# Inverting softmax sums as 128x9 through DRAM, dealing the feed-forward's first steps anew, and storing weight blocks early

## The reference

```python
scores = q @ k.T / 8
bias = -(cum[:, :, :, None] - cum[:, :, None, :])       # cum = cumsum(max(s, 0))
scores = where(causal, -1e9, scores + minimum(bias, 0))
attn = exp(scores - max); attn = attn / (sum(attn) + 1e-9)
x = attn @ v                                            # heads side by side: 576 x 512
h = maximum(x @ w_in, 0)                                # 576 x 1024
conv = three taps along the sequence, per channel
x1 = (h * sigmoid(conv)) @ w_out                        # 576 x 512
u = x1 + (x1.T @ U @ V).T                               # rank 32
out = u + maximum(u @ w_ch1, 0) @ w_ch2                 # 512 -> 2048 -> 512
```

## Time and profile before

| what | value |
|---|---|
| median of three runs | 1002.07 us |
| the profiled execution's own time | 999.37 us |
| its span in the profile | 997.6 us |
| mean granted TensorE clock | 0.971 of full |
| TensorE (PE) busy, matmuls | 929.6 us, 93% |
| VectorE (DVE) busy | 531.9 us, 53% |
| ScalarE (ACT) busy | 350.8 us, 35% |
| DMA queue q1 | 154.66 MB, 49.9% of 16 engines' span |
| chain of work that ended last | PE 75%, DVE 13%, ACT 3%, issue 3%, DMA 2%, SP's issuing 2% |

### The profile page before, as it was taken

How to read it: one execution, slowest core, us unless ns; L and a number is a source line. 1 busy time by engine, 2 the same in 40 slices (tenths; PEclk the granted TensorE clock), 3 DMA queues, 4 the chain that set the end, 5 groups by cost and what they waited for, 6 DMA issues and landing times.

```text
span 997.6 us, 16111 instructions
## 1 busy us (share of the span) xinstructions
PE 929.6 (93%) x6455; PEld 868.0 (87%) x6455; DVE 531.9 (53%) x913; ACT 350.8 (35%) x670; POOL 5.9 (1%) x20
## 2 busy tenths in 40 slices
PE   2898898979999899999999999999999989999998
PEld 1676788968999799987999999987999989889998
DVE  5459896346775583346554784146655670342222
ACT  1365564444333443433332453332332331211111
POOL 1000000000000000000000000000000000000000
PEclk9799997989999799999999999999999999999999
DMA  4677455735564646533645546433555434344441
GB/s 93 137 213 189 110 165 171 214 101 157 179 205 153 180 127 211 191 120 129 186 163 170 169 130 207 154 112 113 177 169 169 170 127 162 127 136 173 167 162 58
DMA packets 68257, 155.68 MB, mean 156 GB/s; under 512 B 30356, under 2 KB 44692, under 8 KB 55896
## 3 DMA queue, kind: packets, MB, share of 16 engines
q1 hardware_dynamic: 68184, 154.66, 49.9%
HBM read 114.57 MB, written 30.03 MB: 145 GB/s over the span
## 4 chain that ended last, share of the span: by engine, by line
PE 75%; DVE 13%; issue 3%; ACT 3%; DMA 2%; SPq 2%; ACTq 0%; DVEq 0%
PE psum L1019 20%; PE psum L1021 18%; PE psum L1020 18%; PE psum L996 8%; PE psum L942 3%; PE psum L975 2%; DVE sums L746 2%; PE psum L973 2%; DVE neg_max L733 2%; DVE work L784 2%; DVE work L787 2%; PE psum L956 1%; DVE work L782 1%; DMA klc<-cum_scratch 1%; DVE ring L844 1%
## 5 line engine op out<-in xcount | busy, mean ns | idle before, releaser
L1019 PE MATMUL psum<-r_hl,ring 128*128 128x288 f32 x512 | 157.7, 308 | 3.8 <-DVE work L816 1.9
L1019 PE MATMUL psum<-uu_hl,ring 128*128 128x288 f32 x512 | 155.8, 304 | 3.1 <-DVE ybuf L806 1.7
L1021 PE MATMUL psum<-r_hl,ring 128*128 128x288 f32 x512 | 152.2, 297 | 0.0
L1020 PE MATMUL psum<-r_hl,ring 128*128 128x288 f32 x512 | 152.2, 297 | 0.0
L1021 PE MATMUL psum<-uu_hl,ring 128*128 128x288 f32 x512 | 151.3, 296 | 0.0
L1020 PE MATMUL psum<-uu_hl,ring 128*128 128x288 f32 x512 | 151.2, 295 | 0.0
L733 DVE TENSOR_REDUCE neg_max<-psum 128x1 f32<-128x512 f32 (+4 forms) x165 | 83.1, 538 | 117.6 <-PE psum L947 110.9
L825 DVE SCALAR_TENSOR_TENSOR r_hl<-psum,r_hl 128x288 fp32r<-128x288 f32 x128 | 58.2, 456 | 154.5 <-ACT r_hl L646 154.3
L996 PE MATMUL psum<-probs,va 128*128 128x320 f32 (+4 forms) x448 | 126.0, 392 | 0.4 <-ACT probs L572 0.4
L646 ACT ACTIVATE r_hl<-psum 128x288 fp32r<-128x288 f32 x128 | 52.4, 411 | 203.8 <-PE psum L1021 203.8
L1019 PEld LDWEIGHTS psum<-r_hl,ring 128*128 128x128 f32 x512 | 97.6, 191 | 7.3 <-DVE work L816 3.1
(11 more groups left out here) (96 smaller groups left out, 1717.4 us busy)
## 6 DMA issues: line engine op xcount, KB each, us to landing
ring<-w_scratch SPq DMA_DIRECT2D x72, 1024.0 KB, 4.9
w_scratch<-ring SPq DMA_DIRECT2D x24, 1024.0 KB, 5.3
kq_raw<-in_kq_t SPq DMA_DIRECT2D x70, 288.0 KB, 4.4
stage<-in_w_ch SPq DMA_DIRECT2D x16, 512.0 KB, 6.7
khc<-khh SPq DMA_DIRECT2D x34, 144.0 KB, 2.3
qm<-qhl SPq DMA_DIRECT2D x34, 144.0 KB, 2.5
out_t<-u_acc SPq DMA_DIRECT2D x16, 288.0 KB, 2.1
va<-in_v SPq DMA_DIRECT2D x34, 128.0 KB, 3.8
```

What stands on the lines that cost most here:

```text
L1019: pe.matmul(o, hi, m_hi, start=start, stop=False)
L1020: pe.matmul(o, hi, m_lo, start=False, stop=False)
L1021: return pe.matmul(o, lo, m_hi, start=False, stop=stop)
```

## The change

It has four parts.

1. **Sums of pairs 0 to 2.** ScalarE evicts one row of sums per head instead of 64 repeated ones. SP gathers the row as 64x9 into `few[0]` (`gather_sums`, at g = 0 of the next head), so that a pair fills 128x9; VectorE inverts it (`invert_few`, at g = 2 of heads 2, 4 and 6, ahead of the low halves of query and key); SP stores it to `few_scratch` (`store_few`, g = 3, behind the load of query and key) and broadcasts it into `spread_out` with two loads (`spread_few`, g = 4); VectorE multiplies on 576 columns (`normalise_few`, at g = 1 of the next head, behind that step's maxima and ahead of the last group). Pair 3 keeps the old way. `sums` has two buffers instead of four, and x is split for pair 2 a step later, at (7, 2).
2. **`order`.** No `up` or `down` pair stands between `wi` pairs any more, and single ones stand between the transposes, `rank` and each `mix` pair.
3. **`spread`.** Beside batch 1's attention, where no older batch is there to fill with, gating, transposes, `rank`, `mix` and the split cost 10 to 12 more each. Batch 0's `wi` then lie in 7 attention steps instead of 9, and its transposes, rank and mix in 9 instead of 3.
4. **Stores.** A block's store is issued two items after the last use of what its place held before, and block 3's right behind batch 0; `store_blocks` is gone.

```diff
+        few_in = Count(sem("few_in"), 32)
+        few_done = Count(sem("few_done"), 1)
+        few_out = Count(sem("few_out"), 16)
+        spread_in = Count(sem("spread_in"), 32)
         recip = Count(sem("recip"), 2)
-        norm = Count(sem("norm"), 1, 4)
+        norm = Count(sem("norm"), 1, 2)
...
-                if f in (4, 7):
-                    fill(1)
...
+            fill(1)
             seq.extend(pair("turn", b, 4))
+            fill(1)
+            seq.extend(pair("rank", b, 0))
             fill(2)
-            seq.extend(pair("rank", b, 0))
-            fill(1)
-            seq.extend(pair("mix", b, 0) + pair("mix", b, 1))
-            fill(1)
-            seq.extend(pair("mix", b, 2) + pair("mix", b, 3))
-            fill(1)
+            for d in range(KT):
+                seq.extend(pair("mix", b, d))
+                fill(1)
             seq.append(("split", b, 0, KT - 1, 0))
-            fill(1)
             assert not late
...
-        def spread(items, steps, idle):
-
-            plan, total, done = [[] for _ in range(idle + steps)], sum(COST[x[0]] for x in items), 0
-            for x in items:
+
+
+        ROUND_TRIP = {"gated": 10, "turn": 12, "rank": 12, "mix": 10, "split": 12}
+
+        def spread(items, steps, idle, alone):
+
+            cost = [COST[x[0]] + (ROUND_TRIP.get(x[0], 0) if alone else 0) for x in items]
+            plan, total, done = [[] for _ in range(idle + steps)], sum(cost), 0
+            for x, c in zip(items, cost):
                 plan[idle + min(done * steps // total, steps - 1)].append(x)
-                done += COST[x[0]]
+                done += c
             return plan
...
+        STORE_AT = {SEQ[AT[before] + 2]: [q] for (b, q), (_, _, before) in BLOCK.items() if b == 0 and before}
...
+        FEW_HEADS = (2, 4, 6)
+        X_SPLIT = {(5, 2): 0, (6, 1): 1, (7, 2): 2}
...
+                def gather_sums(a, h):
+
+                    m, x = a * (NPAIR - 1) + h // 2, h % 2
+                    sp.wait_ge(evict.sem, evict.value(a * H + h))
+                    row = sums[D * (1 - x):D * (1 - x) + 1, h // 2 % 2, :]
+                    sp.dma_start(few[0][x * D:(x + 1) * D, :], row).then_inc(few_in.sem, 16)
+
+                def store_few(a, pair):
+                    sp.wait_ge(few_done.sem, few_done.value(a * (NPAIR - 1) + pair))
+                    sp.dma_start(few_scratch[a * NPAIR + pair].rearrange("x (p c) -> (x p) c", p=D), few[1][:, :])\
+                      .then_inc(few_out.sem, 16)
+
+                def spread_few(a, pair):
+                    m = a * (NPAIR - 1) + pair
+                    sp.wait_ge(few_out.sem, few_out.value(m))
+                    norm.wait(sp, a * NPAIR + pair - 1)
+                    for x in range(2):
+                        row = few_scratch[a * NPAIR + pair][x:x + 1, :]
+                        sp.dma_start(spread_out[x * D:(x + 1) * D, :], row.broadcast_to([D, S])).then_inc(spread_in.sem, 16)
+
                 def attention_step(a, h, g):
+                    if g == 0 and 1 <= h <= 6:
+                        gather_sums(a, h - 1)
                     if g == 2:
                         side(a, h + 2)
                     if g == 3:
                         load(a, h + 3)
+                    if g == 3 and h in FEW_HEADS:
+                        store_few(a, FEW_HEADS.index(h))
+                    if g == 4 and h in FEW_HEADS:
+                        spread_few(a, FEW_HEADS.index(h))
...
-                unstored = list(range(len(WEIGHTS_HEADS) - 1, BLOCKS))
-
-                def store_blocks(last):
-                    while unstored and unstored[0] <= last:
-                        store_block(unstored.pop(0))
-
                 def load_block(b, q):
                     place, nth, before = BLOCK[b, q]
-                    store_blocks(q if b == 1 else -1)
-                    store_blocks(max([x for x in range(BLOCKS) if place_of(x) == place and BLOCK[0, x][1] < nth], default=-1))
                     multiplied(sp, before)
...
-                        else:
-                            store_blocks(q - 1)
-                            if q + 1 < BLOCKS:
-                                load_raw(q + 1)
+                        elif q + 1 < BLOCKS:
+                            load_raw(q + 1)
+                    for q in STORE_AT.get(item, ()):
+                        store_block(q)
...
+                store_block(len(WEIGHTS_HEADS) - 1)
...
-                    norm.wait(act, m - NPAIR)
-                    act.activation(sums[o:o + D, h // 2, :], psf[sm:sm + D, O0:O0 + S], ACT.Identity, bias=EPS).then_inc(evict.sem, 1)
+                    norm.wait(act, m - 2)
+                    if h // 2 < NPAIR - 1:
+                        act.activation(sums[sm:sm + 1, h // 2 % 2, :], psf[sm:sm + 1, O0:O0 + S], ACT.Identity, bias=EPS)\
+                           .then_inc(evict.sem, 1)
+                    else:
+                        act.activation(sums[o:o + D, h // 2 % 2, :], psf[sm:sm + D, O0:O0 + S], ACT.Identity, bias=EPS)\
+                           .then_inc(evict.sem, 1)
                     xl_done.wait(act, m - NPAIR)
...
+                def invert_few(a, pair):
+                    m = a * (NPAIR - 1) + pair
+                    dve.wait_ge(few_in.sem, few_in.value(m))
+                    if m:
+                        dve.wait_ge(few_out.sem, few_out.value(m - 1))
+                    dve.reciprocal(few[1][:, :], few[0][:, :]).then_inc(few_done.sem, 1)
+
+                def normalise_few(a, pair):
+                    x = x_raw[:, pair, :]
+                    evict.wait(dve, a * H + 2 * pair + 1)
+                    dve.wait_ge(spread_in.sem, spread_in.value(a * (NPAIR - 1) + pair))
+                    dve.tensor_tensor(x, x, spread_out[:, :], ALU.mult).then_inc(norm.sem, 1)
+
                 def normalise(a, pair, half):
-                    m = a * NPAIR + pair
-                    x, total = x_raw[:, pair, cols(half)], sums[:, pair, cols(half)]
+
+                    x, total = x_raw[:, pair, cols(half)], sums[:, pair % 2, cols(half)]
                     evict.wait(dve, a * H + 2 * pair + 1)
                     dve.reciprocal(total, total).then_inc(recip.sem, 1)
-                    recip.wait(dve, m, half + 1)
+                    recip.wait(dve, a, half + 1)
                     mul = dve.tensor_tensor(x, x, total, ALU.mult)
...
-                    if g >= 3 and 4 <= h <= 6:
-                        normalise(a, h - 4, g - 3)
+                    if g == 2 and h in FEW_HEADS:
+                        invert_few(a, FEW_HEADS.index(h))
+                    if g == 1 and h - 1 in FEW_HEADS:
+                        normalise_few(a, FEW_HEADS.index(h - 1))
                     if g <= 1 and h == 0 and not first:
                         normalise(a - 1, NPAIR - 1, g)
```

More of the change, by code:

```diff
@@ L79, in attention_and_ffn_program @@
     w_scratch = nc.dram_tensor("w_scratch", (BLOCKS, P, 2 * PIECE), F32, kind="Internal").ap()
+    few_scratch = nc.dram_tensor("few_scratch", (B * H // 2, 2, S), F32, kind="Internal").ap()
     cum_scratch = nc.dram_tensor("cum_scratch", (B * H, 2, S), F32, kind="Internal").ap()
@@ L128, in attention_and_ffn_program @@
         max_split = sb("max_split", [P, NT, P], F32R)
-        sums = sb("sums", [P, NPAIR, S], F32)
+        sums = sb("sums", [P, 2, S], F32)
+        SP9 = S // D
+        few = [sb(f"few{i}", [P, SP9], F32) for i in range(2)]
+        spread_out = sb("spread_out", [P, S], F32)
         x_raw = sb("x_raw", [P, NPAIR, S], F32)
@@ L302, in attention_and_ffn_program @@
                   for a in range(1, B)}
-        PLAN = {a: spread(BESIDE[a], len(ATT_STEPS) - 3 * (a == 1), 3 * (a == 1)) for a in BESIDE}
+        PLAN = {a: spread(BESIDE[a], len(ATT_STEPS) - 3 * (a == 1), 3 * (a == 1), a == 1) for a in BESIDE}
         END = order(B - 1, second(B - 2, UNITS // 2, UNITS)) + flat(second(B - 1, 0, UNITS))
@@ L364, in bodies @@
                         then(a, h, g)
-        X_SPLIT = {(5, 2): 0, (6, 1): 1, (7, 1): 2}
+        FEW_HEADS = (2, 4, 6)
+        X_SPLIT = {(5, 2): 0, (6, 1): 1, (7, 2): 2}
         X_SPLIT_LAST = (0, 2)
```

## The result

The changed kernel took 1016.9 us (median of 4 runs, 1013.59 to 1019.43) against 1000.47 us (4 runs): ratio 1.0159, interval 1.0126 to 1.0192. It is slower by 1.6%; the forecast was slower by 0.6%, and the range ended at 1017 on a median of 1002.07, where the ratio gives 1018. The profiled execution took 1013.59 us with a span of 1011.8, so 14.2 us more than before; the forecast was +7.5.

The account below looks back on a forecast made before the run. TensorE, where it stands still or runs at its lower clock, bounds the kernel. Terms -4.9 + 19.3 + 2.1 + 2 - 3 - 7.1 + 3.4 - 4.5 + 0.2 = +7.5 gave 1008 us, own range 1001 to 1017.

Parts of the forecast that it names:

- What bounds the kernel: Whole kernel: time changes only where TensorE stands still or runs at the lower of its two clocks.
- Batch 0, what goes and comes: Batch 0's six heads: reciprocals leaving give -4.9 us, three DRAM trips +19.3, low clock behind them +2.1.
- The chain: Batch 0, each trip: gather, reciprocal, low halves, load, store, broadcasts and multiply in sequence, delaying the last maxima 6.5 us.
- +2.1: Batch 0's six heads: low clock after the three trips' waits, 0.7 us each.
- Batch 0's feed-forward: Beside batch 1's attention: packing `wi` in 7 steps costs +2 us; spreading transposes, rank and mix gains -3.
- The rival of full cover: Batch 0's feed-forward: attention fully covers the mix steps, gaining 10 us instead of 3, 1001 us in all; chance 17%.
- Early stores: Batch 2: storing block 17 earlier removes a stall and the low clock behind it, -7.1 us.
- +3.4: Batches 2 and 3: eight `wi` pairs without the `down` pair between make the next `down` pair wait, +3.4 us.
- -2.8 and -1.7: Batches 2 and 3: spreading mix pairs removes gaps (-2.8 us) and the low clock stretch at 461.3 (-1.7 us).
- The tail: Tail: the same packing and spreading with less VectorE work beside them, +2 and -1.8, +0.2 us in sum.
- The short trip: Batch 0 trips: transfers land like the quickest loads, maxima 1.8 us late, 992 us in all; chance 18%.
- the clock rival: Batches 2, 3 and tail: packed `wi` brings one more low clock stretch of 3.4 to 6.8 us, 1014 us; chance 13%.

Follow-up runs that it names:

- that edit: Changed kernel with a pair's multiply two steps later, at g = 3 of the next head, behind its maxima: ratio 1.0016.
- single versions above: Changed kernel, six heads: sums stored before load 71.5; gather before weight store 72.3; multiply later 68.5; all three 63.1; plus old order 59.8; weight store back 62.8 us.

## Why the prediction was wrong, point by point

**What bounds the kernel.** Right. TensorE's busy time did not change (929.6 and 930.2); all of the 14.2 us is waits and clock.

**Batch 0, what goes and comes.** The chain was right at every step: the gather behind the weight load, the low halves behind the gather, the store behind the load of query and key, the multiply between the maxima. Landings of 6.3 to 7.0, 4.0 and 3.1 us (the last two medians) stand for the 6.6, 4.5 and 2.3 taken. By the fixed cost that the Trainium skill's page "DMA: Bandwidth & Descriptors", section "Anatomy of one DMA — SWDGE (gpsimd) path", gives, the store would land 2 us after issue; that section fits transfers issued by GpSimd, and this one is issued by SyncE. With nothing of size ahead it took 1.4 and behind the load 4.0, so what stands ahead decides here and not the fixed part. The split of the loss was wrong, and the total came near since two errors cancelled. Six heads took 24.7 us more than six undisturbed ones (6 x 8.9): forecast 21.4, as 19.3 of standing still, over 6 us in each trip, and **+2.1** of clock. The four waits of TensorE in this stretch that the profile shows over 0.3 us (1.50, 1.90, 5.73 and 4.17) make 13.3, and the first of them is for a side load, which the forecast did not have; the other 11 are mostly low clock, which the window shows as 0.82 for 0.97 before. With the 128x9 path alone there is no such side load's wait, the three waits are 6.73, 5.05 and 5.90, 17.7 in all, and 8 us remain for the clock. So its term was four to five times too small. My reason for making it small, that the clock recovers under the next trip's transfers, does not hold: the even head behind a trip has no wait at all and still takes 11.7 us at 0.71 instead of 8.9.

**Batch 0's feed-forward.** Transposes, rank and mix: forecast -3, and +2 for `wi`. Batch 1 fell by 3.0, and by 2.5 with this part alone, where -1 was forecast. The waits came nearly as named, for example 1.06 at 223.96 for a transpose's low half and 1.65 at 239.46 for `mixed`:

```profile
223.96 0.33 PE L1127 MATMUL psum<-ident_f,work 128*128 128x128 f32 x1 [1.06 <-DVE ybuf L859]
...
239.46 0.61 PE L1144 MATMUL psum<-v,ybuf 96*128 96x288 f32 x1 [1.65 <-DVE work L869]
```

Those of the transposes, rank and mix make 5.2 us instead of 6.0, and those beside `wi` 4.9 instead of 5.2, so the +2 did not come. The rest of the gain is the clock: it was low for 10.2 us at the transposes and behind them against 13.6 before, and for 6.8 beside `wi` against 10.2. The rival of full cover (10 us gained) is not borne out.

**Early stores.** Right for this part alone: -7.1 forecast, -10.0 measured, of which 1.7 is the low stretch at 461.3 that the sum had under the mix pairs. But the terms do not add, since the new order by itself also ends the stall; the sum counted the stall's end in full beside it.

**Batches 2 and 3: the step that failed.** The sum had **+3.4** for `wi` and **-2.8 and -1.7** for the spread mix. The waits of batch 3 say otherwise (TensorE, the changed kernel):

```profile
611.53 0.40 PE L1072 MATMUL psum<-r_hl,ring 128*128 128x288 f32 x1 [1.27 <-DVE u_acc L891]
...
657.00 0.40 PE L1072 MATMUL psum<-r_hl,ring 128*128 128x288 f32 x1 [0.98 <-DVE ybuf L859]
...
664.77 0.40 PE L1072 MATMUL psum<-uu_hl,ring 128*128 128x288 f32 x1 [1.73 <-DVE ybuf L859]
...
689.85 0.40 PE L1144 MATMUL psum<-v,ybuf 96*128 96x288 f32 x1 [0.85 <-DVE r_hl L878]
...
715.94 0.40 PE L1072 MATMUL psum<-uu_hl,ring 128*128 128x288 f32 x1 [1.66 <-DVE uu_hl L873]
```

`wi` costs 1.81 (0.54 and 1.27) against 0.29, near the 2.35 forecast for a batch. The transposes and `rank` cost 3.43 against 1.86, a term that the sum did not have at all. Mix and split cost 3.75 (0.85, three of 0.42, 1.66) against 2.10, where 0.7 was expected. I had counted the pairs that the new order puts in and not those that it takes away: two pairs stood ahead of `rank` and one stands there, and behind the split stood one and stands none. By these rows and the smaller ones named, the changed kernel's batch 3 has 4.7 us more of waits, and it became 4.3 longer with the bounds of the earlier trace rows, 4.6 from its head start. The low stretch that the -1.7 was to take out of batch 2 did not go either; another of 3.4 us stands at 433.8, behind a wait of 1.95 us.

**The tail.** +0.2 forecast, -2.5 measured; it had no low stretch, where the one before had two of 3.4 us. No part of the forecast named this, and one execution of each kernel does not show that the change did it.

**The rivals.** None won. The short trip is excluded by the landings; the packed `wi` brought no low stretch to batch 3, so the clock rival's 1014 us, near as it is, has the wrong cause. The chances had slower ahead (0.45). In the profiled executions batches 2 and 3 missed by 8.7 us and batch 0's heads by 3.2, both forecast too low; batch 1 and the tail gave back 2.0 and 2.7, and 0.6 came ahead of head 2.

## What to carry to other kernels

A small transfer's time can be that of what stands ahead of it: here 2.2 us or 7.0 for the same gather. Three trips through DRAM, each to spare VectorE two reciprocals of 1.94 us, cost 20 us where nothing was beside them and nothing where matmuls were. Put the wait for such a trip where its engine has already done what others need: that edit took TensorE's waits from 13.3 to 5.9 us. And when an order of work with a fixed number of fillers is dealt anew, count at each round trip what leaves it, not only what comes.

## What the runs showed of the hardware that was not expected

In batch 0 TensorE waits, in head 3, for the side load of head 4's key (`klc<-cum_scratch`), longer in some traces than in others. With early stores alone this head, from 55.4 to 64.9, took 9.5 us, with a wait of 0.74. With the new costs alone, and the same instructions up to there, the wait was 1.80 us and the window around the head ran at a low clock:

```profile
57.90:72.80 14.90, 13.10 (x63) 10.55 (x62) 5.30 (x11) 5.77 (x10) 0.00 (x0) 0.66 0.39 95
...
61.42 0.79 PE L947 MATMUL psum<-khc,qm 68*128 68x512 f32 x1 [1.80 <-DMA klc<-cum_scratch]
```

That is 5 to 6 us for a wait under 2. Nine of the kernels here have the old sums, and so the same instructions in batch 0's six heads. These took 58.2 to 60.4 us in four traces, where the wait was 0.74 us or less, and 65.5 to 65.8 in five, where it was 1.35 to 1.80 and 10.2 us at the low clock followed. The wait of 2.47 us behind the reciprocals, which all nine have, came with no low stretch in two traces, with one of 3.4 us in one and with one of 6.8 us in six:

```profile
52.60:110.80 58.20, 52.51 (x374) 42.34 (x373) 44.20 (x72) 34.07 (x60) 0.00 (x0) 1.00 0.71 190
...
48.80:114.30 65.50, 59.31 (x374) 48.09 (x373) 45.23 (x73) 34.07 (x60) 0.00 (x0) 0.87 0.63 169
```

The first row is of the new order alone, the second of the one with the four mix pairs spread.

25 runs of the kernel before spread from 990.85 to 1004.54 us, in which the granted clock went from 0.983 for the shortest to 0.968 for the longest. A part of a change that is worth 2 us is hard to tell from the whole time here. In batches 2 and 3 the windows of its stage tell it, with their waits; in batch 0's heads a window of one trace does not, since the same instructions differ by 7 us. So the six heads of single versions above (71.5, 72.3, 68.5, 63.1, 59.8 and 62.8 us) can be told from the changed kernel's 78.1 only with their waits and their ratios beside them, and hardly from each other.
